# A gated scan and an ELU feed-forward layer on one core: the 512-column products visit the columns of a row in four passes

## The chip, the core and the metric

The kernel runs on one of the cores of a Trainium2 chip. A core has TensorE (PE, matrix products; its weight loads have a row of their own, PEld), VectorE (DVE), ScalarE (ACT), GpSimd (POOL) and SyncE (SP), which here issues most transfers. Each engine works through its own list of instructions in order, and semaphores tie the lists together. The metric is the device time of one execution in microseconds, the median of three runs; lower is better.

## The reference

```python
sig = 1.0 / (1.0 + np.exp(-f_logit))
f = lower_bound + (1.0 - lower_bound) * sig          # per channel
h = f[:, t] * h + (1.0 - f[:, t]) * x[:, t]          # scan over t; y[:, t] = h
# y: (2, 6080, 256), seen as 12160 tokens of 256
h = y @ w_in                                         # 256 -> 2048
g = np.where(h > 0.0, h, np.exp(np.minimum(h, 0.0)) - 1.0)
out = g @ w_out                                      # 2048 -> 256
```

All inputs and the output are float32.

## The kernel before, in words

Channels lie on the 128 partitions and tokens along the row. The 6080 tokens of each of the two batches are cut into 12 blocks: a first one of 448 tokens (`SHORT`) and eleven of 512 (`TILE`), and both batches of a block are worked on together. A block of one batch and one unit of 128 hidden channels is a tile of 128 x 512 numbers; a block has 2 x 16 = 32 such tiles.

**Products.** Every float32 operand is split into a rounded part (`_hi`, type fp32r) and a rest (`_lo`), and each product is made of three matmuls that add up in one bank of PSUM: hi x hi, hi weights x lo data, lo weights x hi data. The first layer of the blocks from the second on works on pairs of units (`q` from 0 to 7) and pairs of batches by a seven-product scheme (P1 to P7, Strassen's kind, with sums and differences prepared beforehand): seven products give the four tiles C11, C12, C22, C21 of a pair. Function `product` issues one of them (lines 855, 857, 859). Function `second` issues the second layer's product of one tile and one half of the 256 outputs (lines 886, 887, 888), which adds into the bank `acc` over all 16 units. The first block has its own functions for the first layer (`first_products`, `first_product`, lines 958 to 993) without the seven-product scheme, and uses `second` with 448 columns.

**Order.** The order on every engine is written out by hand. On TensorE a block from the second on is function `whole`: eight rounds (one for each `q`) of 15 products: P1, P5, two halves of an older C21, P2, P6, both halves of C11, one of C12, P3, P7, the other half of C12, both of C22, P4. That is 7 + 8 products, 45 matmuls a round. Between products TensorE waits on semaphores: for `fork_ready` (ACT copies the bank of P1 for a second use, line 449), `u4_ready` and `c22_ready` (DVE adds two PSUM banks with a saved P5, lines 696 and 704), `g_ready` (DVE has finished a tile's ELU, line 710), and `g_lo_ready` (POOL has made the rest of a finished tile, line 327). ACT makes Relu and Exp of each tile (lines 457 and 463) and rounds it (line 471). Scan, gates and sums of the block that follows are spread over the rounds on DVE, ACT and POOL. SP reloads and stores with waits on the same semaphores.

**Warm-up.** Before the first product TensorE runs 18 matmuls of bf16 zeros with 512 columns (line 999).

**Operands of a matmul.** Data is read as `bank[:, 0:w]`, `a_h[:, 0:w]` and so on, that is, `w` numbers of four bytes next to each other in each partition, and the bank is written in the same order. Weights are 128 x 128 blocks that are loaded anew for each matmul.

Of the kernel before, what the change touches and what calls it, by code (L numbers as in the profile page):

```python
# [23 lines left out]
RING = 8  # L24
LEAD = 6
OPEN = 6
WARM_UP = 18
EDGE = 8

WIDE = 1  # L30

# [15 lines left out]

QUARTER = ((P1, P5), (P2, P3))
PLACE = ((P1, P2), (P5, P4))


def width(j):
    return SHORT if isinstance(j, int) and j == 0 else TILE
# [18 lines left out]
def gated_scan_elu_ffn(nc, first_gate, forget_logit, value, w_in, w_out, out):  # L72
    ctx = ExitStack()
    with ctx:
        def sb(name, shape, dt=F32):
            return ctx.enter_context(nc.sbuf_tensor(name, shape, dt))
# [25 lines left out]

        sb("room_of_edge", [P, P - EDGE])
        opening = sb("opening", [P, EDGE + BATCH * HALVES * TILE])
        gate = opening[:, EDGE:].rearrange("p (b i t) -> p b i t", b=BATCH, i=HALVES)
        bound = opening[:, EDGE - HALVES:EDGE]
        x = sb("x", [P, BATCH, HALVES, TILE])
# [11 lines left out]
        g_hi = sb("g_hi", [P, RING, TILE], F32R)  # L119
        g_lo = sb("g_lo", [P, RING, TILE], F32R)  # L120
# [69 lines left out]
        def a_parts(par, product):  # L190
            if product == P4:
                return a4_hi[:, :], a4_lo[:, :]
            k = product
            return a_hi[:, par, k], a_lo[:, par, k]

        def y(b, i, w):
            return x[:, b, i, 0:w]
# [16 lines left out]
        def _(sp):  # L214
# [4 lines left out]
            def load_x(j, b, i):  # L219
                sp.dma_start(x[:, b, i, 0:width(j)],  # L220
                             value[b, :, i, tokens(j)]).then_inc(x_loaded[b][i], 16)
# [7 lines left out]
            def reload_first():  # L229
                for b in range(BATCH):  # L230
# [4 lines left out]
                    for i in range(HALVES):  # L235
                        sp.wait_ge(a_lo_ready[PLACE[b][i]], 1)
                        load_x(1, b, i)
# [31 lines left out]

            sp.dma_start(opening[:, EDGE - HALVES:EDGE + SHORT], first_gate).then_inc(gate_loaded[0][0], 16)  # L270
            load_x(0, 0, 0)
# [137 lines left out]
        def _(act):  # L409
# [19 lines left out]
            def split_first(b, i):  # L429

                act.wait_ge(scan_ready, HALVES * b + i + 1)
                nc.scalar.copy(a_parts(0, PLACE[b][i])[0][:, 0:SHORT], y(b, i, SHORT)).then_inc(a_hi_ready, 1)

# [416 lines left out]
        def _(pe):  # L850
            def product(j, par, q, k, bank, start=False):
                w = width(j)
                hi, lo = w_in_hi[:, q, k], w_in_lo[:, q, k]
                a_h, a_l = a_parts(par, k)
                nc.tensor.matmul(bank[:, 0:w], hi, a_h[:, 0:w], start=start, stop=False,  # L855
                                 skip_group_check=True)
                nc.tensor.matmul(bank[:, 0:w], hi, a_l[:, 0:w], start=False, stop=False,  # L857
                                 skip_group_check=True)
                return nc.tensor.matmul(bank[:, 0:w], lo, a_h[:, 0:w], start=False, stop=True,  # L859
                                        skip_group_check=True)  # L860

            def second(j, t, half):

                w = width(j)
                first = isinstance(j, int) and j == 0
                if first:
                    b, unit = FIRST_TILES[t]
                    opens = unit == 0
                else:
                    b, unit = TILE_OF[t % TILES][0], 2 * (t // TILES) + TILE_OF[t % TILES][1]  # L870
                    opens = unit == b
                q, u = divmod(unit, 2)
                closes = unit == UNITS - 1 - b
                if half == 0:
                    if first:
                        pe.wait_ge(w_out_lo_ready[q], 1)
                    if opens and first and b == 1:

                        pe.wait_ge(g_ready, max(k for k in range(TILES * PAIRS) if FIRST_BANK[k] >= TILES) + 1)
                    if opens and not first:  # L880
                        pe.wait_ge(acc_copied, BATCH * HALVES * (j - 1) + HALVES * (b + 1))
                    pe.wait_ge(g_lo_ready, TILES * PAIRS * j + t + 1)
                cols = slice(half * P, (half + 1) * P)
                hi, lo = w_out_hi[:, q, u, cols], w_out_lo[:, q, u, cols]
                bank = acc[:, b, half, 0:w]
                nc.tensor.matmul(bank, hi, g_hi[:, t % RING, 0:w], start=opens, stop=False)  # L886
                nc.tensor.matmul(bank, hi, g_lo[:, t % RING, 0:w], start=False, stop=False)  # L887
                done = nc.tensor.matmul(bank, lo, g_hi[:, t % RING, 0:w], start=False, stop=closes)  # L888
                if half == 1:
                    done.then_inc(mm2_done, 1)  # L890
                elif closes:
                    done.then_inc(acc_half, 1)

            def whole(j, par):
                def m(q, back, i, half):

                    at = q - back
                    if at >= 0:
                        second(j, TILES * at + i, half)
                    else:  # L900
                        second(j - 1, TILES * (PAIRS + at) + i, half)

                for q in range(PAIRS):
# [7 lines left out]
                    else:  # L911
                        pe.wait_ge(g_ready, TILES * (n - 2) + C21 + 1)
                    product(j, par, q, P1, trunk(q), start=True).then_inc(p1_done, 1)
                    if q == 0:
                        pe.wait_ge(a_lo_ready[P5], low_count(j, P5))
                    pe.wait_ge(g_ready, TILES * (n - 1) + C12 + 1)
                    product(j, par, q, P5, h[:, 2], start=True).then_inc(p5_done, 1)
                    m(q, 2, C21, 0)
                    m(q, 2, C21, 1)
                    if q == 0:  # L920
                        pe.wait_ge(a_lo_ready[P2], low_count(j, P2))
                    pe.wait_ge(fork_ready, n - PAIRS + 1)
                    product(j, par, q, P2, h[:, 3]).then_inc(c11_ready, 1)
                    if q == 0:
                        pe.wait_ge(a_lo_ready[P6], low_count(j, P6))
# [19 lines left out]
            def plain_weights(unit, half):  # L945
                p, u = divmod(unit, 2)
                k = QUARTER[half][u]
                return w_in_hi[:, p, k], w_plain_low[p][:, k]

            def first_products():  # L950

                pieces = [a_parts(0, PLACE[0][i]) for i in range(HALVES)]
                pe.wait_ge(zeros_ready, 3)
# [22 lines left out]
            def first_product(t):  # L976
# [6 lines left out]
                for half in range(HALVES):  # L983
                    pe.wait_ge(a_lo_ready[PLACE[b][half]], 1)
                    hi, lo = plain_weights(unit, half)
                    a_h, a_l = [part[:, 0:SHORT] for part in a_parts(0, PLACE[b][half])]
                    if t == TILES * PAIRS - 2 and half == 0:
# [9 lines left out]
            zeros = e[:, 0].bitcast(mybir.dt.bfloat16)  # L997
            for k in range(WARM_UP):
                nc.tensor.matmul(h[:, k % 4, :], zeros[:, 0:P], zeros[:, 0:TILE], start=True, stop=True)  # L999
            first_products()  # L1000
            for t in range(OPEN, TILES * PAIRS):
                first_product(t)
                if t >= LEAD:
                    for half in range(HALVES):
                        second(0, t - LEAD, half)
# [46 lines left out]
```

## Time and profile before

| | us |
|---|---|
| median of 3 runs | 989.86 |
| all three runs | 989.86, 989.53, 2022.61 |
| span of the profiled execution, first to last instruction | 987.9 |
| busy of TensorE in it | 983.2 |

The profiled execution's own time is not listed apart from the runs; its span is 2.0 us under the median. The third run took about twice as long; the trace is not of it.

How to read it: the profile page gives, for each engine, the sum of busy time; matmuls overlap in the records (each one's modelled end lies behind the start of the next), so a row's duration of a matmul is longer than the distance between two. That distance, from start to start, is what a matmul costs on TensorE when it never waits, and it is read from the timeline or from counts in windows.

### The profile page before, as it was taken

The page shows a single profiled execution, that of the slowest core. Times are in us where ns is not written, and L with a number is a line of the kernel's source. Part 1 is how long each engine was busy: PE and PEld are TensorE (multiplying, and loading weights), DVE is VectorE, ACT ScalarE, POOL GpSimd, SP SyncE. Part 2 cuts the span into 40 slices and gives each one's busy share as a digit, 9 for nine tenths or more (in the row PEclk, how much of TensorE's full clock was granted, in tenths as well). Part 3 has the DMA queues.
Part 4 walks back from the last instruction along what each step waited for, and adds up shares of the span by engine and source line. Part 5 has one row for each costly group of instructions (what it writes and reads, how often), then busy time and mean ns, then how long its engine had stood idle before and what let it go on. Part 6 is the DMA issues. An engine that isn't in the chain of part 4 may idle for free.

```text
span 987.9 us, 15016 instructions
## 1 busy us (share of the span) xinstructions
PE 983.2 (100%) x4362; PEld 817.7 (83%) x4362; DVE 726.4 (74%) x916; ACT 791.6 (80%) x1424; POOL 633.2 (64%) x477
## 2 busy tenths in 40 slices
PE   9999999999999999999999999999999999999998
PEld 6998888888888888888888888888888888888887
DVE  6987876976886796697688679678768867956444
ACT  7988878878888887877887887888788788787775
POOL 2588796576567558557656756856765765675444
PEclk9999999999999999999999999999999999999999
DMA  7212012002102201200210210120021021001001
GB/s 265 66 33 91 0 35 63 33 1 76 54 1 60 69 1 42 64 21 10 65 53 0 64 63 0 51 66 10 25 61 42 0 74 53 0 0 45 1 1 43
DMA packets 23078, 42.02 MB, mean 43 GB/s; under 512 B 2560, under 2 KB 4096, under 8 KB 23040
## 3 DMA queue, kind: packets, MB, share of 16 engines
q1 hardware_dynamic: 22752, 41.10, 12.9%
q10 hardware_dynamic: 288, 0.46, 0.1%
q8 instruction: 18, 0.29, 0.1%
q14 instruction: 20, 0.16, 0.1%
HBM read 29.10 MB, written 12.45 MB: 42 GB/s over the span
## 4 chain that ended last, share of the span: by engine, by line
PE 100%; DVE 0%; POOL 0%; issue 0%; POOLq 0%
PE acc L886 17%; PE acc L888 17%; PE acc L887 17%; PE h L859 14%; PE h L855 14%; PE h L857 14%; PE h L992 1%; PE h L993 1%; PE h L991 1%; PE h L999 1%; PE h L958 0%; PE h L968 0%; PE acc L991 0%; PE acc L992 0%; PE acc L993 0%; PE acc L958 0%
## 5 line engine op out<-in xcount | busy, mean ns | idle before, releaser
L327 POOL TENSOR_TENSOR g_lo<-e,g_hi 128x512 fp32r<-128x512 f32 (+1 forms) x384 | 519.4, 1363 | 348.6 <-ACT g_hi L471 347.7
L457 ACT ACTIVATE e<-h 128x512 f32<-128x512 f32 (+1 forms) x379 | 225.6, 595 | 151.7 <-PE h L859 129.2
L710 DVE SCALAR_TENSOR_TENSOR e<-e,h 128x512 f32<-128x512 f32 (+1 forms) x379 | 256.3, 676 | 70.7 <-ACT e L463 70.4
L887 PE MATMUL acc<-g_lo,w_out_hi 128*128 128x512 f32 (+1 forms) x768 | 297.2, 387 | 0.0
L886 PE MATMUL acc<-g_hi,w_out_hi 128*128 128x512 f32 (+1 forms) x768 | 297.2, 387 | 0.0
L888 PE MATMUL acc<-g_hi,w_out_lo 128*128 128x512 f32 (+1 forms) x768 | 297.2, 387 | 0.0
L463 ACT ACTIVATE e<-e 128x512 f32<-128x512 f32 (+1 forms) x384 | 241.5, 629 | 9.6 <-issue 1.2
L471 ACT CAST g_hi<-e 128x512 fp32r<-128x512 f32 (+1 forms) x384 | 232.4, 605 | 16.9 <-DVE e L710 16.9
L859 PE MATMUL h<-a_hi,w_in_lo 128*128 128x512 f32 x616 | 239.7, 389 | 0.0
L855 PE MATMUL h<-a_hi,w_in_hi 128*128 128x512 f32 x616 | 239.7, 389 | 0.0
L857 PE MATMUL h<-a_lo,w_in_hi 128*128 128x512 f32 x616 | 239.6, 389 | 0.0
L887 PEld LDWEIGHTS acc<-g_lo,w_out_hi 128*128 128x128 f32 x768 | 144.2, 188 | 28.5
L888 PEld LDWEIGHTS acc<-g_hi,w_out_lo 128*128 128x128 f32 x768 | 144.2, 188 | 28.4
L886 PEld LDWEIGHTS acc<-g_hi,w_out_hi 128*128 128x128 f32 x768 | 144.2, 188 | 28.4
L859 PEld LDWEIGHTS h<-a_hi,w_in_lo 128*128 128x128 f32 x616 | 115.7, 188 | 24.1
L857 PEld LDWEIGHTS h<-a_lo,w_in_hi 128*128 128x128 f32 x616 | 115.7, 188 | 23.9
L855 PEld LDWEIGHTS h<-a_hi,w_in_hi 128*128 128x128 f32 x616 | 115.7, 188 | 23.8
L704 DVE TENSOR_TENSOR h<-p,h 128x512 f32<-128x512 f32 x88 | 61.0, 693 | 77.7 <-PE h L859 77.4
L619 DVE TENSOR_TENSOR_SCAN x<-opening,carry,x 128x512 f32<-128x512 f32 (+1 forms) x48 | 102.6, 2138 | 0.1
L689 DVE COPY p<-h 128x512 f32<-128x512 f32 x88 | 59.7, 678 | 50.6 <-PE h L859 50.5
L696 DVE TENSOR_TENSOR h<-p,h 128x512 f32<-128x512 f32 x88 | 60.7, 689 | 37.4 <-PE h L859 35.6
L611 DVE SCALAR_TENSOR_TENSOR x<-opening,x 128x512 f32<-128x512 f32 (+1 forms) x48 | 57.4, 1196 | 0.1
(77 smaller groups left out, 563.0 us busy)
## 6 DMA issues: line engine op xcount, KB each, us to landing
opening<-forget_logit SPq DMA_DIRECT2D x44, 256.0 KB, 2.6
x<-value SPq DMA_DIRECT2D x44, 256.0 KB, 2.7
out<-out_sb SPq DMA_DIRECT2D x44, 256.0 KB, 2.0
w_in_raw<-w_in SPq DMA_DIRECT2D x8, 256.0 KB, 6.1
w_out_raw<-w_out SPq DMA_DIRECT2D x8, 256.0 KB, 6.8
out<-out_sb SPq DMA_DIRECT2D x4, 224.0 KB, 1.9
x<-value SPq DMA_DIRECT2D x3, 224.0 KB, 6.6
opening<-forget_logit SPq DMA_DIRECT2D x2, 224.0 KB, 6.6
```

The lines of the kernel that those rows point to most:

```text
L327: nc.gpsimd.tensor_tensor(g_lo[:, t % RING, 0:w], e[:, t % TILES, 0:w], g_hi[:, t % RING, 0:w].bitcast(F32), ALU.subtract).then_inc(g_lo_r ...
L457: nc.scalar.activation(e[:, i, 0:w], bank_of(j, t)[:, 0:w], ACT.Relu, scale=-1.0).then_inc(r_ready, 1)
L463: nc.scalar.activation(e[:, t % TILES, 0:w], e[:, t % TILES, 0:w], ACT.Exp, scale=-1.0).then_inc(e_ready, 1)
L471: nc.scalar.copy(g_hi[:, t % RING, 0:w], e[:, t % TILES, 0:w]).then_inc(g_hi_ready, 1)
L619: nc.vector.tensor_tensor_scan(x[:, b, i, 0:w], gate[:, b, i, 0:w], x[:, b, i, 0:w], carry[:, b, i], ALU.mult, ALU.subtract).then_inc(scan ...
L710: nc.vector.scalar_tensor_tensor(e[:, t % TILES, 0:w], e[:, t % TILES, 0:w], -1.0, bank_of(j, t)[:, 0:w], ALU.add, ALU.max).then_inc(g_rea ...
L855: nc.tensor.matmul(bank[:, 0:w], hi, a_h[:, 0:w], start=start, stop=False, skip_group_check=True)
L857: nc.tensor.matmul(bank[:, 0:w], hi, a_l[:, 0:w], start=False, stop=False, skip_group_check=True)
L859: return nc.tensor.matmul(bank[:, 0:w], lo, a_h[:, 0:w], start=False, stop=True, skip_group_check=True)
L886: nc.tensor.matmul(bank, hi, g_hi[:, t % RING, 0:w], start=opens, stop=False)
L887: nc.tensor.matmul(bank, hi, g_lo[:, t % RING, 0:w], start=False, stop=False)
L888: done = nc.tensor.matmul(bank, lo, g_hi[:, t % RING, 0:w], start=False, stop=closes)
```

## The change

A helper `in_order` views the columns of a row as 32 blocks of 4 groups of 4 columns (with 512 columns), and walks over them with the group's place in the block as the outermost loop: first columns 0 to 3, 16 to 19, 32 to 35 and so on, then 4 to 7, 20 to 23 and so on, in four passes. The data read and the PSUM bank written of a matmul both get this view, so column n of the data still ends in column n of the bank. It is used for all matmuls of `product` and for those of `second` outside the first block. The first block's matmuls, the warm-up, the weights, all other engines, the order of the instructions and all waits are as they were; each engine's list has as many rows as before.

```diff
+LINE = 4
+APART = 4
...
+def in_order(columns):
+
+    return columns.rearrange("p (b a c) -> p a b c", a=APART, c=LINE)
...
                 a_h, a_l = a_parts(par, k)
-                nc.tensor.matmul(bank[:, 0:w], hi, a_h[:, 0:w], start=start, stop=False,
-                                 skip_group_check=True)
-                nc.tensor.matmul(bank[:, 0:w], hi, a_l[:, 0:w], start=False, stop=False,
-                                 skip_group_check=True)
-                return nc.tensor.matmul(bank[:, 0:w], lo, a_h[:, 0:w], start=False, stop=True,
-                                        skip_group_check=True)
+                into = in_order(bank[:, 0:w])
+                a_h, a_l = in_order(a_h[:, 0:w]), in_order(a_l[:, 0:w])
+                nc.tensor.matmul(into, hi, a_h, start=start, stop=False, skip_group_check=True)
+                nc.tensor.matmul(into, hi, a_l, start=False, stop=False, skip_group_check=True)
+                return nc.tensor.matmul(into, lo, a_h, start=False, stop=True, skip_group_check=True)
...
                 bank = acc[:, b, half, 0:w]
-                nc.tensor.matmul(bank, hi, g_hi[:, t % RING, 0:w], start=opens, stop=False)
-                nc.tensor.matmul(bank, hi, g_lo[:, t % RING, 0:w], start=False, stop=False)
-                done = nc.tensor.matmul(bank, lo, g_hi[:, t % RING, 0:w], start=False, stop=closes)
+                g_h, g_l = g_hi[:, t % RING, 0:w], g_lo[:, t % RING, 0:w]
+                if not first:
+                    bank, g_h, g_l = in_order(bank), in_order(g_h), in_order(g_l)
+                nc.tensor.matmul(bank, hi, g_h, start=opens, stop=False)
+                nc.tensor.matmul(bank, hi, g_l, start=False, stop=False)
+                done = nc.tensor.matmul(bank, lo, g_h, start=False, stop=closes)
```

## Rows read from the trace of the kernel before

**Rows 1.** The page: busy time, share of the span, instructions of each engine.
```profile
PE 983.2 (100%) x4362; PEld 817.7 (83%) x4362; DVE 726.4 (74%) x916; ACT 791.6 (80%) x1424; POOL 633.2 (64%) x477
```
**Rows 2.** Waits of TensorE: engine, line, releaser: us in total, times, longest.
```profile
PE h L999 <- POOL e L384: 1.3, 1, 1.3
PE h L958 <- issue: 0.2, 1, 0.2
```
**Rows 3.** Windows: start:end, length, busy (instructions) of each engine, granted clock, DMA, GB/s.
```profile
core 0: us, PE busy (x) PEld busy (x) DVE busy (x) ACT busy (x) POOL busy (x), PEclk, DMA share, GB/s
300.00:500.00 200.00, 200.00 (x884) 165.66 (x883) 146.44 (x184) 161.91 (x288) 129.85 (x98) 1.00 0.14 44
```
**Rows 4.** Groups by line and shape on TensorE: count, busy us, mean ns, idle before.
```profile
L886 PE MATMUL acc<-g_hi,w_out_hi 128*128 128x512 f32 x704 | 273.9, 389 | 0.0
L859 PE MATMUL h<-a_hi,w_in_lo 128*128 128x512 f32 x616 | 239.7, 389 | 0.0
```
**Rows 5.** Timeline of TensorE, 512 columns: start us, duration us, line, tiles.
```profile
500.39 0.39 PE L886 MATMUL acc<-g_hi,w_out_hi 128*128 128x512 f32 x1
500.62 0.39 PE L887 MATMUL acc<-g_lo,w_out_hi 128*128 128x512 f32 x1
...
503.11 0.39 PE L886 MATMUL acc<-g_hi,w_out_hi 128*128 128x512 f32 x1
```
**Rows 6.** Timeline of TensorE, first block, 448 columns.
```profile
16.30 0.36 PE L991 MATMUL h<-a_hi,w_in_hi 128*128 128x448 f32 x1
...
18.73 0.36 PE L991 MATMUL h<-a_hi,w_in_hi 128*128 128x448 f32 x1
```
**Rows 7.** Timeline of the weight loads in the warm-up (bf16, 512 columns), late and early.
```profile
6.78 0.10 PEld L999 LDWEIGHTS h<-e 128*128 128x128 bf16 x1 [0.21 <-issue]
...
7.00 0.10 PEld L999 LDWEIGHTS h<-e 128*128 128x128 bf16 x1
...
7.22 0.10 PEld L999 LDWEIGHTS h<-e 128*128 128x128 bf16 x1
...
7.43 0.10 PEld L999 LDWEIGHTS h<-e 128*128 128x128 bf16 x1
...
2.15 0.15 PEld L999 LDWEIGHTS h<-e 128*128 128x128 bf16 x1 [0.27 <-issue]
2.58 0.15 PEld L999 LDWEIGHTS h<-e 128*128 128x128 bf16 x1 [0.28 <-issue]
```
**Rows 8.** Line 999 and line 859 by themselves: duration ns min/median/max, first and last start.
```profile
L999 PE MATMUL h<-e x18: 379/634/634, 1.3 to 7.6; 128*128 128x512 bf16 x18
...
L859 PEld LDWEIGHTS h<-a_hi,w_in_lo x616: 187/188/188, 81.0 to 977.3; 128*128 128x128 f32 x154
L859 PE MATMUL h<-a_hi,w_in_lo x616: 389/389/398, 81.2 to 977.5; 128*128 128x512 f32 x154
```
**Rows 9.** Timeline of all engines at the end of a round: P7's last matmul to P4.
```profile
505.60 0.39 PE L859 MATMUL h<-a_hi,w_in_lo 128*128 128x512 f32 x1
...
506.13 0.70 DVE L704 TENSOR_TENSOR h<-p,h 128x512 f32<-128x512 f32 x1 [0.40 <-PE h L859]
...
507.87 0.39 PE L855 MATMUL h<-a_hi,w_in_hi 128*128 128x512 f32 x1
```
**Rows 10.** Longest waits for TensorE: engine, line, releaser: us in total, times, longest.
```profile
ACT e L457 <- PE h L859: 129.2, 248, 1.1
DVE h L704 <- PE h L859: 77.4, 68, 2.1
```

## The prediction, made before the changed kernel ran

> **What bounds the kernel now.** I read the busy shares first. TensorE is busy for 983.2 of 987.9 us and its weight loads for 83%, no other engine for more than 80% [rows 1]. Busy can still hide waiting, so the second view is TensorE's waits: 1.5 us in all, both before the first real product [rows 2]. From there to the end it runs one matmul behind another. The other engines wait for it instead, ACT for 129.2 us and DVE for 77.4 us on line 859 alone [rows 10]. So the time is a number of matmuls times the distance between their starts, and only those two can matter.
>
> The distance is not the 389 ns of the duration column, since matmuls overlap. In the timeline twelve matmuls of 512 columns take 503.11 - 500.39 = 2.72 us [rows 5], 226.7 ns each. Over a longer stretch, 884 matmuls touch 200 us [rows 3], 226.2 ns; this count includes the ones cut by the window's edges, so I take 226.7. The granted clock there is 1.00 [rows 3], which is 2.4 GHz: 512 columns need 213.3 ns, and 226.7 ns are 544 cycles. A matmul thus takes **32 cycles, 13.3 ns, more than its columns**. That excess is the only thing in this kernel that a different walk over the same columns could take away.
>
> **What the change touches.** Of the 4362 matmuls, those of lines 886, 887, 888 with 512 columns are 3 x 704, and those of lines 855, 857, 859 are 3 x 616 [rows 4]: 3960 together, at 226.7 ns 897.6 us, 91% of the span. The rest, first block, warm-up and tail, 90 us, keeps its instructions. No instruction is added, moved or removed, no wait either, and bytes read and written are the same. So the sum has one unknown, the change x of the distance, and 3960 x is the result. 1 ns is worth 3.96 us; 2% of the time (about what a measurement of this kernel can tell from no change) is 19.8 us, or 5.0 ns, 12 cycles a matmul.
>
> **The unknown from both sides.** The trace before has no matmul with a broken walk, so no row prices one.
> - Best end: the whole excess goes. x = -13.3 ns, 3960 x 13.3 = 52.8 us, 937 us. A column a cycle can't be beaten.
> - A nearer row on the good side: late in the warm-up the weight loads of bf16 matmuls with 512 columns start at 6.78, 7.00, 7.22 and 7.43 [rows 7], 217 ns apart, and the shortest record of that line is 379 ns against 389 for the fp32r ones [rows 8]. Both say 10 ns less for the same number of columns, into the same kind of bank, with a weight load for each as well. So most of the excess belongs to the four-byte operands, and not to PSUM or to the passing from one matmul to the next as such. What differs for four bytes is the data's read, twice the bytes a column, and the weight load, which takes 188 ns against 100 [rows 8, 7]. The first is what the walk changes.
> - Middle: x = 0.
> - Bad end: each of the 128 steps from one group of four to a group that doesn't adjoin it costs a cycle of 0.42 ns. x = 53.3 ns, 211 us, 1201 us. The farthest row is a matmul at half the rate, the early bf16 ones, 0.43 us apart [rows 7]: x = +203 ns, 804 us, near 1794 us.
>
> I take x = -10.0 ns, the distance of the bf16 matmuls: the nearest row, and a distance that this array has shown for 512 columns; of the two things that differ between the bf16 and the fp32r matmuls, the read of the data is the one that is needed in each cycle of the 544, while the weight load has 39 ns to spare. 3960 x 10.0 = 39.6 us; 987.9 - 39.6 = **948.3 us of span**. The median stands 2.0 us over the span of the profiled execution, which gives **950 us**. The Trainium skill ("TensorE: Matmul & The Clock Gate", Wait — 56ns, not 53.3ns?) gives 215.7 ns for a warm 512-column matmul; the trace's late bf16 rows agree within their rounding of 10 ns, and with that figure the estimate would be 946 us.
>
> **What else stands behind TensorE.** If TensorE gets faster, something may become late. Per round of 45 matmuls, 10.20 us, ACT works 161.91 / 200 of it, 8.26 us, DVE 7.5 and POOL 6.6 [rows 3]; a round of 9.75 us still leaves ACT 1.5 us. The tight places are where TensorE needs a sum built from its own last result: P7's last matmul starts at 505.60, DVE's addition ends at 506.83 and P4 starts at 507.87 [rows 9], 1.04 us of slack with nine matmuls between. Ten distances, each 10 ns shorter, take 0.1 us off that. ACT and DVE wait for TensorE more than the reverse, so these lists shift with it. I cost this at nothing. The weight load comes sooner to its limit: 188 ns, started when the matmul before starts. In the first block with 448 columns the distance is (18.73 - 16.30) / 12 = 202.5 ns [rows 6], 15.8 ns over its 186.7 ns of columns, more than the 13.3 ns over for 512. I read this as the weight load's chain (188 ns and some 14 more) ruling there. It would allow anything down to 202.5 ns with 512 columns, so it doesn't cap the gain.
>
> **Rivals.**
> 1. *Nothing happens, 990 us.* The excess is fixed per fp32r matmul: the swap to four-byte weights, or a cost of the weight load's reads that doesn't care for the data's order. For it: TensorE's lines of 512 columns have one and the same mean of 389 ns whichever tile is read [rows 4], whatever the other engines do meanwhile; and the excess with 448 columns is not smaller than with 512 [rows 5, 6], as one per column would be (11.7 ns), unless the weight load hides it. Against it: the bf16 rows also load weights each time and have 10 ns less. Chance 0.25. A broken walk that is neither helped nor hurt lands here too.
> 2. *Slower: the breaks cost.* Place: the read of the data or the add into PSUM, which now jumps by 64 bytes after every four columns, 128 times a matmul, where before it never did. Price: 0.42 ns per break that costs a cycle, 1201 us if all do. It decides from 12 cycles, one break in 11, since TensorE has no slack at all to hide them [rows 2]. For it: nothing in the trace shows that a break is free, and a memory read ahead in blocks of more than 16 bytes would be wasted now. Against it: each group of four is still 16 adjoining bytes on both sides. [...] Chance 0.19, most of it at 1100 us and more.
> 3. *More: the whole excess goes, 937 us.* It would need the handover between matmuls to be free too, against the late bf16 rows. Chance 0.05.
> 4. *Half of it: about 970 us.* Either 5 ns a matmul go (3960 x 5 = 20 us), or 10 go and half comes back as waits at P2, P3 and P4. Against the second: the slack above. Chance 0.05.
>
> **How the numbers follow.** The forecast has the rest, 0.46. Faster by over 2% (below 970): forecast, rival 3 and rival 4, 0.56 in all. Within 2%: rival 1, 0.25. Slower: rival 2, 0.19. The range from 936 to 998 holds all but the slower case: its low end is the floor of one cycle a column, its high end leaves 8 us over rival 1 for a walk that costs up to 5 cycles a matmul. The forecast's own range, with the distance between 213.3 and 219 ns, is 936 to 960.
>
> **What would show it.** In the profile of the changed kernel: the groups of 512 columns on TensorE at 379 ns and not 389, and twelve starts in 2.60 us, not 2.72, with the first block's 202.5 ns and the weight loads' 188 ns as before. TensorE's waits should stay at 1.5 us; if P2, P3 or P4 wait for ACT or DVE, rival 4 is at work. 226.7 ns again means rival 1; anything from 232 ns on means rival 2, and then the waits of ACT and DVE for TensorE grow. A distance that differs between the lines of `product` and of `second` would mean that not the walk but the place of the operands decides, and would make this working wrong in its root.

## The result: 1.3% faster, a third of the forecast gain

| | median us | all runs |
|---|---|---|
| before | 989.75 | 989.53 to 989.86, one of 2022.61 left out of the comparison |
| changed | 976.52 | 976.29 to 977.58 (4) |
| changed / before | 0.9869 | 95% interval 0.9854 to 0.9883 |

The profiled execution of the changed kernel took 976.51 us, with a span of 974.6. The gain is 13.2 us and clear of noise, but within 2%. The forecast was 950 us, from 10.0 ns less per matmul.

The page's shares, to be read beside [rows 1], and TensorE's waits, beside [rows 2]:

```profile
PE 969.0 (99%) x4362; PEld 815.1 (84%) x4362; DVE 724.4 (74%) x916; ACT 790.7 (81%) x1424; POOL 630.6 (65%) x477
```
```profile
PE h L1010 <- POOL e L393: 1.3, 1, 1.3
PE h L969 <- ACT a_hi L441: 1.1, 1, 1.1
```

TensorE bounds the kernel as before. Its only waits, 2.4 us in all, stand at the warm-up and the first product; from there it never waits, so the whole gain is in the distance between matmuls. The window that [rows 3] showed, and the groups of [rows 4], in the changed kernel:

```profile
300.00:500.00 200.00, 200.00 (x897) 167.62 (x896) 150.47 (x189) 164.53 (x294) 130.03 (x98) 1.00 0.15 47
```
```profile
L897 PE MATMUL acc<-g_hi,w_out_hi 128*128 128x512 f32 x704 | 270.4, 384 | 0.0
...
L868 PE MATMUL h<-a_hi,w_in_lo 128*128 128x512 f32 x616 | 236.6, 384 | 0.0
...
L897 PE MATMUL acc<-g_hi,w_out_hi 128*128 128x448 f32 x64 | 23.4, 365 | 0.0
```

897 matmuls touch the 200 us and not 884. The lines of `second` and of `product` fell alike, 389 to 384 ns, and the first block's 448-column groups stayed at 365. The timeline of TensorE (start, duration), to be read beside [rows 5], shows something that an average hides:

```profile
494.88 0.38 PE L866 MATMUL h<-a_hi,w_in_hi 128*128 128x512 f32 x1
495.11 0.38 PE L867 MATMUL h<-a_lo,w_in_hi 128*128 128x512 f32 x1
495.32 0.39 PE L868 MATMUL h<-a_hi,w_in_lo 128*128 128x512 f32 x1
495.56 0.39 PE L866 MATMUL h<-a_hi,w_in_hi 128*128 128x512 f32 x1
495.78 0.38 PE L867 MATMUL h<-a_lo,w_in_hi 128*128 128x512 f32 x1
...
497.56 0.38 PE L897 MATMUL acc<-g_hi,w_out_hi 128*128 128x512 f32 x1
```

Twelve distances take 497.56 - 494.88 = 2.68 us, 223.3 ns each, 536 cycles of 2.4 GHz where there were 544. But they are no longer equal. From the nanosecond starts in the trace they run 230, 224, 221, 218 ns, over and over, whatever line or tile comes: a rhythm of four. Before, every one from 130 us on was 226 or 227. 3960 x 3.33 ns = 13.2 us, which is the measured gain.

### The profile page after: what moved, and what is told of

It is laid out like the page before. It is cut to its first block, busy times and chain, and to the rows that moved or that the text cites. A ratio compares the mean times of both kernels' runs of the same rounds, so it can differ in the third digit from the quotient of the medians.

```text
span 974.6 us, 15016 instructions
## 1 busy us (share of the span) xinstructions
PE 969.0 (99%) x4362; PEld 815.1 (84%) x4362; DVE 724.4 (74%) x916; ACT 790.7 (81%) x1424; POOL 630.6 (65%) x477
## 4 chain that ended last, share of the span: by engine, by line
PE 99%; DMA 0%; DVE 0%; ACT 0%; issue 0%; DVEq 0%
PE acc L898 17%; PE acc L897 17%; PE acc L899 17%; PE h L868 14%; PE h L867 14%; PE h L866 14%; PE h L1004 1%; PE h L1003 1%; PE h L1002 1%; DMA opening<-first_gate 0%; PE h L969 0%; PE h L979 0%; PE acc L1002 0%; PE acc L1003 0%; PE acc L1004 0%; DVE x L628 0%
## 5 line engine op out<-in xcount | busy, mean ns | idle before, releaser
L897 PE MATMUL acc<-g_hi,w_out_hi 128*128 128x512 f32 (+1 forms) x768 | 293.7, 382 | 0.0
L898 PE MATMUL acc<-g_lo,w_out_hi 128*128 128x512 f32 (+1 forms) x768 | 293.7, 382 | 0.0
L899 PE MATMUL acc<-g_hi,w_out_lo 128*128 128x512 f32 (+1 forms) x768 | 293.7, 382 | 0.0
L866 PE MATMUL h<-a_hi,w_in_hi 128*128 128x512 f32 x616 | 236.6, 384 | 0.0
L868 PE MATMUL h<-a_hi,w_in_lo 128*128 128x512 f32 x616 | 236.6, 384 | 0.0
L867 PE MATMUL h<-a_lo,w_in_hi 128*128 128x512 f32 x616 | 236.5, 384 | 0.0
```

Of the source, the lines that this page charges most:

```text
L866: nc.tensor.matmul(into, hi, a_h, start=start, stop=False, skip_group_check=True)
L867: nc.tensor.matmul(into, hi, a_l, start=False, stop=False, skip_group_check=True)
L868: return nc.tensor.matmul(into, lo, a_h, start=False, stop=True, skip_group_check=True)
L897: nc.tensor.matmul(bank, hi, g_h, start=opens, stop=False)
L898: nc.tensor.matmul(bank, hi, g_l, start=False, stop=False)
L899: done = nc.tensor.matmul(bank, lo, g_h, start=False, stop=closes)
```

## The experiments

The theories. **A**: the data's read collides with the weight load of the next matmul, and the order of reads changes that. **B**: the add into PSUM is what is relieved. **C**: it is the timing against the other engines. **D**: a fixed cost of a four-byte matmul, from which the walk takes 8 cycles. **E**, formed after the fifth run: how data and weights stand to each other, in place and in time, decides the excess, so a walk has more than one self-keeping rhythm.

In the kernels that run TensorE alone, each group of 40, 48 or 64 matmuls has its own line, start and stop flags set and four banks in turn unless said; operands start on a multiple of 256 bytes unless said. The cuts of these kernels stand here in short form, with names written out. "Distance" is the mean distance between a group's starts in the trace, its first eight left out.

### Walks, columns and shifts, TensorE alone, and the walk on one side only

```diff
+for k in range(64):
+    matmul(bank(k), W(k), D(k), start=True, stop=True)                        # plain
+for k in range(64):
+    matmul(bank(k), W(k), passes(D(k), 4, 4), start=True, stop=True)          # data only
+for k in range(64):
+    matmul(passes(bank(k), 4, 4), W(k), D(k), start=True, stop=True)          # bank only
```

> TensorE alone: 39 groups of 64 matmuls, each group with its own form, nothing else running on the other engines; the output is only a copy of a piece of x. Quantity read: mean distance between starts in each group. Before and after had 226.7 and 223.3 ns with four-byte operands. Theory A (the data's read and the weight load for the next matmul meet in the memory): walking only the data in four passes gives 223 ns, walking only the bank 226.7; bf16 stays at 216 with any walk; the distance moves when the data or the weights are shifted by 16 or 32 bytes against each other. Theory B (the add into PSUM is what is relieved): walking only the bank gives 223, only the data 226.7, and shifts do nothing. Theory C (the excess is fixed per four-byte matmul and the walk changes something else of the kernel, its timing against the other engines): all walks of 512 columns here give the same distance. On columns: with a fixed excess of 13.3 ns, 448 columns give 200 and 256 give 188 + 14 = 202 because of the weight load; with one cycle for each 16 columns, 480 give 212.5.

| group, 128 weight columns | distance ns | cycles |
|---|---|---|
| 512 columns, plain | 226.7 | 544 |
| four passes on data and bank | 223.4 | 536 |
| four passes on the data only | 223.4 | 536 |
| four passes on the bank only | 226.7 | 544 |
| data in 2 passes / 8 passes of groups of 4 | 231.1 / 246.7 | 555 / 592 |
| data in 4 passes, groups of 2 / of 8 / of 16 | 461.4 / 230.7 / 239.5 | 1107 / 554 / 575 |
| 480, 384, 320, 256 columns, plain | 216.7, 173.3, 146.7, 120.0 | 520, 416, 352, 288 |
| 448 columns, plain / in four passes | 202.7 / 197.3 | 486 / 474 |
| plain, data 16 / 32 / 64 bytes on | 231.6 / 233.3 / 228.9 | 556 / 560 / 549 |
| plain, weights 16 bytes on | 233.3 | 560 |
| one bank for all, or adding | 226.7 | 544 |
| bf16, plain (the usual distance, two records are missing) / four passes | 216 / 228.9 | 518 / 549 |

Rows of three groups: duration ns min/median/max, first and last start.

```profile
L75 PE MATMUL h<-d,w x64: 379/384/390, 63.1 to 77.2; 128*128 128x512 f32 x64
...
L77 PE MATMUL h<-d,w x64: 389/389/398, 77.4 to 91.7; 128*128 128x512 f32 x64
...
L117 PEld LDWEIGHTS h<-d,w x64: 187/192/192, 420.9 to 428.5; 128*128 128x128 f32 x64
L117 PE MATMUL h<-d,w x64: 281/283/283, 421.0 to 428.6; 128*128 128x256 f32 x64
```

Line 75 (data only) has the 384 ns of the changed kernel, line 77 (bank only) the 389 of before, so B falls; nothing else ran, so C falls. Line 117 has 256 columns and starts a matmul every (428.6 - 421.0) / 63 = 121 ns (120.0 from the nanosecond starts) although each weight load's record is 192 ns long: a chain of weight loads does not set the distance at 202.5 ns, as the prediction had it. The excess is 32 cycles with 256, 320 and 384 columns as with 512 (and 36 to 40 with 416, 448, 480 and 496), so it isn't one per column, and it moves when the data or the weights move by 16 bytes. Most walks lose; in groups of 2 the distance doubles. A missed one thing: bf16 in four passes of groups of 4 did not stay at 216 ns but took 228.9, so two-byte data has an excess of its own when its order is broken up. In groups of 8 columns, 16 bytes as with fp32r, it had 215.8 (in the kernel that follows).

The two halves of the change in the whole kernel:

```diff
-                into = in_order(bank[:, 0:w])
+                into = bank[:, 0:w]
...
-                    bank, g_h, g_l = in_order(bank), in_order(g_h), in_order(g_l)
+                    g_h, g_l = in_order(g_h), in_order(g_l)
```

> The changed kernel with the walk in four passes on the data alone; the banks are written in plain order, so the columns of a product land permuted (the numbers are not the reference's, the work is the same). Theory A (data read against weight load): 976.5 us as with both, distance 223.3 ns. Theory B (PSUM): 989.8 us, distance 226.7 ns. Theory C: 976.5 if any walk does it.

```diff
-                a_h, a_l = in_order(a_h[:, 0:w]), in_order(a_l[:, 0:w])
+                a_h, a_l = a_h[:, 0:w], a_l[:, 0:w]
...
-                    bank, g_h, g_l = in_order(bank), in_order(g_h), in_order(g_l)
+                    bank = in_order(bank)
```

> The changed kernel with the walk on the banks alone; the data is read in plain order, so the columns land permuted (the numbers are not the reference's, the work is the same). Theory A: 989.8 us, distance 226.7 ns. Theory B: 976.5 us, distance 223.3 ns.

Data only: 976.43 us (ratio 0.9863, 0.9847 to 0.988). Bank only: 989.81 us (1.0, 0.999 to 1.001). The window of 300 to 500 us of the first, then of the second:

```profile
300.00:500.00 200.00, 200.00 (x897) 167.65 (x896) 150.85 (x189) 164.48 (x293) 129.98 (x98) 1.00 0.15 47
```
```profile
300.00:500.00 200.00, 200.00 (x884) 165.61 (x883) 146.49 (x183) 161.85 (x288) 129.91 (x98) 1.00 0.14 44
```

The read of the data is all of the gain. PSUM is indifferent to this walk.

### Fewer weight columns, and the first block too

```diff
+for k in range(64):
+    matmul(bank(k)[0:16], W(k)[:, 0:16], D(k), start=True, stop=True)         # also 96, 64, 32
```

> TensorE alone again, groups of 64 matmuls, the output a copy of a piece of x. Plain order had 544 cycles (226.7 ns) for 512 columns and 32 cycles more than its columns for 480, 384, 320 and 256 columns, so the excess isn't per data column. Theory A (the data's read meets the weight load of the next matmul, and gives way): the excess goes with the number of weight columns, 32 cycles with 128, 24 with 96, 16 with 64, 8 with 32; in ns 226.7, 223.3, 220, 216.7; in four passes 223.3, 220.8, 218.3, 215.8. Theory D (a fixed cost per four-byte matmul, of the handover): 226.7 ns with every number of weight columns, and the four passes save the same 8 cycles each time. Shifts: if only the place of data and weights relative to each other counts, shifting both by the same amount gives 226.7 again; if each has to start on a 64-byte boundary for itself, 231 or more. Data shifted by 16, 32 or 64 columns in four passes: 223.3 for whole 64 bytes by both.

| weight columns | 128 | 96 | 64 | 32 | 16 |
|---|---|---|---|---|---|
| plain, ns | 226.7 | 230.0 | 230.0 | 231.7 | 231.7 |
| four passes, ns | 226.7 | 233.3 | 216.7 | 222.9 | |

```profile
L79 PEld LDWEIGHTS h<-d,w x64: 94/94/98, 92.5 to 107.1; 128*16 128x16 f32 x64
L79 PE MATMUL h<-d,w x64: 391/395/397, 92.7 to 107.3; 128*16 128x512 f32 x64
```

(The text on record counts 480 columns among those with 32 cycles over; it has 40.) Neither theory holds. With an eighth of the weights in plain order the load's record halves to 94 ns and the distance grows to (107.3 - 92.7) / 63 = 232 ns, so the excess is not a toll per weight read (A as first put), nor is it fixed (D). In four passes it goes up with 96 weight columns and down with 64, to 216.7 ns. Plain order with data and weights shifted alike gave 230.0 (4 columns), 226.7 (8) and 226.7 (16), so the difference of the two starts counts for much but not for all. And the group of four passes with 128 weight columns, the very form that had 223.4 ns, had 226.7 here. Its distances ran 226, 220, 221, 221, 234, 239, 225: another rhythm, of seven. In the same kernel four passes with the weights 256 bytes on gave 223.4 again, and with the data 64 bytes on 220.0, constant. Very short matmuls behave differently: 128 columns took 213.3 ns in plain order, more than 256 columns do, beside weight loads with records of 333 ns, and 111.6 ns in four passes.

The second kernel of this pair walks the first block's matmuls in four passes as well, 347 of its 384 (the few that open it stay plain):

```diff
-                if not first:
-                    bank, g_h, g_l = in_order(bank), in_order(g_h), in_order(g_l)
+                bank, g_h, g_l = in_order(bank), in_order(g_h), in_order(g_l)
...
-                        nc.tensor.matmul(bank, hi, a_h, start=half == 0, stop=False)
+                        nc.tensor.matmul(in_order(bank), hi, in_order(a_h), start=half == 0, stop=False)
```

(and its two sister lines in `first_product`)

> The changed kernel with the four passes in the first block's 402 or so matmuls of 448 columns too (lines of first_product and second). Alone, 448 columns took 202.7 ns in plain order and 197.4 ns in four passes. Theory A with those sizes: 400 x 5.3 ns = 2.1 us less than the changed kernel, 974.4 us, 0.9847 of before. The reading in the prediction that the weight load's chain rules at 448 columns: no change from 976.5 us.

Measured: 988.46 us (0.9987, 0.9978 to 0.9996), twelve more than the changed kernel, in each of 11 runs (987.78 to 988.89). The long stretch's code is untouched by this edit. Its timeline:

```profile
499.10 0.38 PE L896 MATMUL acc<-g_hi,w_out_hi 128*128 128x512 f32 x1
499.32 0.38 PE L897 MATMUL acc<-g_lo,w_out_hi 128*128 128x512 f32 x1
499.54 0.38 PE L898 MATMUL acc<-g_hi,w_out_lo 128*128 128x512 f32 x1
499.76 0.39 PE L866 MATMUL h<-a_hi,w_in_hi 128*128 128x512 f32 x1
500.00 0.40 PE L867 MATMUL h<-a_lo,w_in_hi 128*128 128x512 f32 x1
500.23 0.39 PE L868 MATMUL h<-a_hi,w_in_lo 128*128 128x512 f32 x1
500.46 0.39 PE L866 MATMUL h<-a_hi,w_in_hi 128*128 128x512 f32 x1
500.69 0.38 PE L867 MATMUL h<-a_lo,w_in_hi 128*128 128x512 f32 x1
```

Seven distances from 499.10 to 500.69 are 1.59 us, 227 ns each, 220 to 240 apart: the rhythm of seven, from 100 us on to the end. The first block did get faster, as the 448-column group alone had said (199.3 ns a matmul from 16.3 to 79 us, against 202.8). Then the stretch behind it started at another moment, fell into the slow rhythm and kept it for some 3900 matmuls, 3.33 x 3900 = 13.0 us, less the 1.2 us that the first block gained. That refutes D and is what E was formed on. One rival stays with this pair alone: both ran on another chip than the kernels above, and no run of the changed kernel is on record for that chip. The kicks below vary the history on one chip.

### Kicks and starts, TensorE alone, and 64 bytes in the kernel

```diff
+matmul(bank(0)[:, 0:200], W(0), D(0)[:, 0:200], start=True, stop=True)        # the kick
+for k in range(48):
+    matmul(passes(bank(k), 4, 4), W(k), passes(D(k, shift=52), 4, 4), start=True, stop=True)
```

> TensorE alone, groups of 48 matmuls in four passes with the data's start 0, 4, ... 60 columns on, each after one of four kicks that change the moment at which the group starts: none, one matmul of 200 columns, three of 360, one of bf16. The output is a copy of a piece of x. Seen so far in four passes without a shift: 223.3 ns (a rhythm of four distances, 230, 224, 221, 218) and, after another history, 226.7 ns (a rhythm of seven, 220, 221, 221, 234, 239, 225, 226). Theory E (the excess is where the data's read and the weights' read stand to each other in time when they meet, which the walk and the start of the matmul decide together): the unshifted groups show 223.3 after some kicks and 226.7 after others, plain order stays at 226.7 after all. Theory D (fixed cost, and the walk just saves 8 cycles): 223.3 after every kick. With the data 16 columns (64 bytes) on: 220.0 after every kick if that rhythm is the only one there, a second value if not.

> TensorE alone, groups of 40 matmuls in four passes, with the weights' start 4, 8 or 12 columns on and the data's 0 to 60; then 448 columns with the data 0 to 28 on. The output is a copy of a piece of x. Theory E: the distance depends on both starts; the best value known is 220.0 ns (data 16 on, or weights 12 on), and a few places near 216 are possible, since 64 weight columns gave 216.7. If only the difference of the two starts counted, weights 12 on with data 12 on would be 223.3 or 226.7.

| four passes, weights on a multiple of 256 bytes | ns after the kicks tried |
|---|---|
| data 0 on | 223.4 (none, bf16), 226.7 to 227.0 (200 columns, three of 360) |
| data 16 columns on | 223.4 to 223.9 (all four), 220.0 in the kernel before this one |
| data 12, 24 or 28 on | 222 to 225, 225 to 232, 222 to 228 |
| data 52 on | 220.0, 220.0 |
| plain, data 0 on | 226.7 to 226.9 (all four) |

E holds as far as history goes: one and the same form has two values on one chip, and which one depends on what ran ahead of it. That a single matmul can decide isn't shown here yet, since the group ahead of the kick differed too (plain order before "none", shifted data before the others). The expectation of one value for 16 columns on failed. Moving the weights as well (the second kernel) gave 220.0 wherever the data starts 12 columns (48 bytes) short of the weights, modulo 64 columns: (weights, data) = (4, 56), (8, 60), (12, 0), beside (0, 52). With (4, 48) it was 240.0. No place came near the 216 ns hoped for. So mostly the difference of the two starts counts, though (4, 20) and (12, 36), with other differences, had 220.0 too.

In the whole kernel, 64 bytes (16 columns) ahead of the data, with the walk and in plain order:

```diff
+        sb("step", [P, 16])
         a_hi_at = -(-nc.sbuf_base // 32) * 32
```

> The changed kernel with 64 unused bytes ahead of the split data, so that all data that TensorE reads starts 64 bytes later; weights stay. Theory E with the 220.0 ns seen alone: 3960 x (223.3 - 220.0) = 13.2 us less than the changed kernel, 963.3 us, 0.973 of before. Theory D: no change, 976.5 us. If a slower rhythm is met in the kernel: 976 to 990 us.

> The kernel before, in plain order, with the same 64 unused bytes. Alone, plain order with the data 64 bytes on had 228.9 ns. Theory E: 3960 x 2.2 = 9 us more than before, 998.8 us. Theory D: 989.8 us.

With the walk 975.71 us (0.9858, 0.9841 to 0.9874): the long stretch ran 222, 225, 221, 225 ns, a third rhythm with the mean 223.3 of the changed kernel, and not the 220.0 one, so my 963.3 failed. In plain order 997.69 us (1.0079, 1.0063 to 1.0096), against 998.8 expected: the place of the data alone costs 8 us.

### The place that all starts lead to

The 52 columns are 208 bytes, so the split data went into one tile whose first 52 columns stay free:

```diff
+STEP = 52
...
+        rows = 4 * (PRODUCTS - 1) + 2 + 2 * RING
+        data = sb("data", [P, STEP + rows * TILE], F32R)[:, STEP:].rearrange("p (r t) -> p r t", r=rows)
+        first, last = 2 * (PRODUCTS - 1), 4 * (PRODUCTS - 1)
+        a_hi = data[:, 0:first].rearrange("p (s k) t -> p s k t", s=2)
+        a_lo = data[:, first:last].rearrange("p (s k) t -> p s k t", s=2)
+        a4_hi, a4_lo = data[:, last], data[:, last + 1]
+        g_hi, g_lo = data[:, last + 2:last + 2 + RING], data[:, last + 2 + RING:]
```

> The changed kernel with all data that TensorE reads in one tile that leaves 52 columns (208 bytes) free at its start, so that data starts 208 bytes past a multiple of 256 and weights on one. Alone, four passes with the data 52 columns on had 220.0 ns from both kicks tried, one constant distance. Theory E: 3960 x (223.3 - 220.0) = 13.2 us less than the changed kernel, 963.3 us, 0.973 of before. Theory D (8 cycles off a fixed cost): 976.5 us. If the kernel's history leads to another rhythm: 976 to 990.

> The same with four passes in the first block too, whose 448-column matmuls come before the others and so change how the long stretch starts; without the 208 bytes that change of history cost 12 us. Theory E with a rhythm at 208 bytes that all histories end in: 963.3 us, less up to 2 us of the first block. If that place has a second rhythm as well: 970 to 990 us.

> TensorE alone, groups of 48 matmuls, the output a copy of a piece of x: plain order with the data 4 to 60 columns on; four passes with the data 52 on after seven kicks and unshifted after three more; 448 columns in four passes; other walks at 16, 32 and 52 columns on; fewer weight columns at 52. Theory E: plain order has no start with less than 226.7 ns except perhaps at 52, since there the plain walk meets the weights' lines as it does anywhere; data 52 on in four passes 220.0 after every kick; unshifted 223.3 after some and 226.7 after others. Theory D: everything in four passes 223.3.

208 bytes on: **963.61 us** (0.9736, 0.972 to 0.9752). With the first block in four passes too: **962.24 us** (0.9722, 0.9706 to 0.9738), its four runs (962.03 to 962.35) all below the other's (963.36 to 964.07). Both beat before and the change. Timeline of the first of them:

```profile
499.46 0.38 PE L865 MATMUL h<-data,w_in_hi 128*128 128x512 f32 x1
499.68 0.38 PE L866 MATMUL h<-data,w_in_hi 128*128 128x512 f32 x1
499.90 0.38 PE L867 MATMUL h<-data,w_in_lo 128*128 128x512 f32 x1
...
502.10 0.38 PE L896 MATMUL acc<-data,w_out_hi 128*128 128x512 f32 x1
```

Twelve distances in 2.64 us, each 220.0 ns, 528 cycles. In the second, whose first block leads up to it differently, the same 220.0 stands from 130 us to the end: the two histories that differed by 12 us before now lead to one rhythm. Alone, the place gave 220.0 after all seven kicks (one of them none), while unshifted data gave 223.4 after one more kick and 226.6 and 227.0 after two. The groups with 223.4 and 226.6 are neighbours of one form, with nothing between them but one matmul of 300 columns: a single matmul can change the rhythm. Plain order never got below 226.7 in 16 starts (60 columns on also had 226.7, the others 229 to 235; at 52 it had 234.6, so my "perhaps at 52" was wrong). Four passes in groups of 8 with the data 52 on also had 220.0; no walk tried with 128 weight columns was better.

## Why the prediction was wrong, step by step

- **What bounds the kernel: right.** TensorE never waits after the first product, and each ns of distance was worth 3.96 us: 3.33 ns and 13.2 us. The long stretch had 223.3 ns and durations of 384, between the 226.7 and 389 of before and the 216.7 and 379 that the forecast named.
- **Where the excess sits: right in kind.** The bf16 rows pointed to the four-byte operands and away from PSUM; the walk on the data alone gave the whole gain and the walk on the bank nothing.
- **The size: wrong, and this is the step that failed.** I took x = -10.0 ns from the bf16 rows [rows 7, 8] and it was -3.3. The bf16 distance is a bound on what is lost by four-byte operands, and I priced the change as if the walk cured all of it. The walk took 8 cycles off on average, of the 26 between the two kinds. Even the best place found took 16 of them (528 cycles). Between rival 1 (nothing, 0) and the forecast I had one case, half of it, at 0.05, and a forecast's own range of 213.3 to 219 ns that left out 219 to 225. The time lay between rival 4 (970) and rival 1 (990), where I had put almost nothing. The wide range of 936 to 998 holds it, and holds four of the five cases.
- **That it came out faster at all: in part luck.** Nothing in the working foresaw that one walk has several rhythms. With the first block walked too, the same long stretch had 226.7 ns and the gain over before was 1.2 us.
- **The weight load's chain at 448 columns: wrong.** [rows 6] were read as a limit of 202.5 ns; 256 columns ran at 120 ns with the same loads, and 448 in four passes at 197.3. The 38 cycles over 448 columns fall with the walk of the data as the 32 over 512 do.
- **Nothing comes late behind TensorE: right.** At 223.3 and at 220.0 ns no wait of TensorE for ACT, DVE or POOL appeared after the first product. Rival 4's waits did not come.
- **Rival 2, the breaks cost: wrong for this walk, right for its neighbours.** Groups of 4 in four passes pay nothing, but 8 passes cost 20 ns, and groups of 2 cost 235. The Trainium skill ("PSUM — Partial Sum Buffer", Specifications) says that any access pattern that isn't contiguous slows matmuls significantly; here the bank's broken walk in groups of 4 was free (226.7 ns alone, ratio 1.0 in the kernel), and groups of 2 on the bank were not tried. What decides is on the data's side. There the Trainium skill ("SBUF — State Buffer", Door 1: The DMA port swizzle, the note on cachelines) asks for at least two hits in each 16-byte line for full bandwidth; this agrees only in part, since groups of 2 make two hits and doubled the distance.
- **Rival 1's argument that equal distances mean a fixed cost: wrong.** The constant 226.7 belonged to one order and one place: in plain order with the data 64 bytes on it was 228.9, with the walk 208 bytes on 220.0.
- **The sign for "the place of the operands decides": blind.** I would have seen it in a difference between the lines of `product` and of `second`. They fell alike, to 384 ns, because in this kernel all data and weights start on multiples of 512 bytes; the place decides all the same, as the shifts showed.

**What stays open.** How the excess arises. The runs show that it depends on the walk over the data, on the starts of data and weights modulo 256 bytes, on the number of weight columns and on what ran ahead of a stretch, and not on the bank's walk. That reads of data and weights get in each other's way is a guess that the shifts suggest and no run shows: fewer weight columns made the excess larger in plain order, and no run had a four-byte matmul without a weight load. Which history leads to which rhythm can't be told ahead.

## What to carry to other kernels

Where one engine never waits, read the distance between its starts over some tens of instructions from the timeline, not the duration column and not the mean alone: its pattern shows what a mean hides. A faster mode seen elsewhere in the trace bounds a gain; it doesn't say how much of the gap an edit closes, and the likeliest case deserves a range from zero to the bound. Before an order of reads is kept, try it after several different starts and with its operands in several places: here the same code was worth 13 us, 1 us or, with 208 free bytes, 26 us.

## What the runs showed that I had not expected

- A deterministic stretch of matmuls can keep one of several rhythms for over 800 us: four distances with a mean of 223.3 ns or seven with 226.7, for the same instructions. What ran before chooses: one matmul between two groups of one form was enough.
- 16 bytes of shift in the data's or the weights' start cost 5 to 7 ns of 226.7 in plain order. In the kernel before, all of both start on a multiple of 512 bytes, which is one of the two best places of plain order that were tried.
- Reading four-byte data in groups of two columns doubles the distance, to 461 ns; reading every eighth 16 bytes costs 20 ns, every fourth gains 3.
- A weight load's record can be longer than the distance between matmuls (192 against 120 ns, with 256 columns), so its length alone is no bound on the rate.
